# Clustered attention before two feed-forward networks: preparation of the heads rewritten, with copies by DMA and part of the one-hot arithmetic on GpSimd

## The chip, the cores and the metric

One core of a Trainium2 chip runs the whole program. The metric is the device time in microseconds, from the first to the last instruction with what the launch puts around it; lower is better. The engines are named as in the profile: PE is TensorE (matmuls), PEld its weight loads, DVE is VectorE, ACT is ScalarE, POOL is GpSimd, SP is SyncE, which here only issues DMAs.

## The reference

Two batches of eight heads, 768 positions of width 64, and 16 cluster centres a head. A query may attend to a key only if both are nearest, by cosine, to the same centre.

```
q_assign = argmax(q_n @ c_n.T);  k_assign = argmax(k_n @ c_n.T)      # first of equal ones
scores   = where(q_assign == k_assign, q @ k.T / 8, -1e9)
attn     = softmax(scores) @ v                                       # 16 heads of 768 x 64
x        = attn, heads side by side                                  # 1536 tokens x 512
h = x @ w1_in;  g = P(h) / (Q(h) + 1e-6);   x2  = g @ w1_out         # P cubic, Q quadratic, 2048 wide
h = x2 @ w2_in; g = h - tanh(h);            out = g @ w2_out
```

Everything is float32. TensorE is fed numbers rounded to a shorter form (F32R), and each product of weight is made of a rounded part (hi) and its rest (lo): hi x hi, hi x lo, lo x hi.

## The kernel before

The 768 queries of a head are six tiles of 128; the sixteen heads give 96 tiles (`TILES`). Each engine has its own list of work, with semaphores between them.

For one tile, in order: `score_tile` (PE, L945) makes 128 x 768 scores in two PSUM banks, in two accumulating parts, ka with qa (the hi and lo halves of q against hi of k) and kb with qb (hi of q against lo of k, and 16 rows that hold the one-hot of the query's cluster against the mask of the key's cluster times a huge number). `row_max` (DVE, L731) takes the largest, `exp_tile` (ACT, L502) the exponential and its sum, `row_sum` and `row_inverse` (DVE, L736 and L743) its inverse, `scale_probs` (POOL, L349) multiplies. `transpose_probs` (PE, L957) turns the tile in six 128 x 128 pieces into two banks (`pt_ps`), `pt_high` (ACT, L509) and `pt_low` (DVE, L749) split it into hi and lo, and `values` (PE, L968) multiplies with v for three tiles at a time (384 queries, a half of a head). ACT copies one half of the result's partitions beside the other (`other_half`, L592), DVE adds (`add_halves`, L831), ACT and POOL make x_hi and x_lo.

Beside it the next heads are prepared. POOL splits q and k into hi and lo (`nat_q`, `nat_k`) and v (`split_v`, L377); `unit` (PE) is a piece of the preparation: three transposes from nq_a, nk or nq_b into the bank pr_ps (L939), or twelve matmuls with the centres (L929, the similarities). There are nine units a head, eight of them transposes, 24 in all: q, k in the order hi and lo, k in the order hi and hi, and q once more with the one-hot beside it. ACT copies each out (L494, L496, L497). DVE turns the similarities into a one-hot (`onehot`, L705 to L725): sum, maximum, equal to the maximum, times a rank, maximum, equal.

The order of the work is written by hand. `section(s, ...)` is six steps, one tile each, and `STEP_UNITS` says which unit goes with which step; a loop (`Fori`) runs over pairs of heads on every engine, with register-valued waits on SP and POOL. Scores run three tiles ahead of the transposes; there are two score buffers and three of probabilities. The first two heads are prepared ahead of the loop (`FIRST_UNITS`). SP issues all DMAs.

The feed-forward networks follow in 96 steps: `hidden(n)` (PE, L1014) and `output(n)` (L1035) of twelve matmuls each, `tile1` or `tile2` on ACT and DVE, `g_low` on POOL (L462). Weights come in chunks of 512 KB, are rounded by ACT (`round_weights`, L519) and split by POOL (L392) or DVE (L777). Chunks 0 to 3 are loaded at the start of the program, 4 and 5 after the last scores, the others when the attention's memory is free. The first three hidden steps stand between the last tiles of the attention.

Of the kernel before, what the change touches and what calls it, by code (L numbers as in the profile page):

```python
# [5 lines left out]
def clustered_attention_then_two_ffns(  # L6
# [32 lines left out]
    PAIRS = HEADS // 2  # L39
    T = S // P  # L40
# [15 lines left out]
    MASK_AT = 96  # L56
    LANES = 4
    TILES = HEADS * T
    DURING = 6
# [14 lines left out]
    with ctx:  # L74
# [32 lines left out]
        raw_v = [sb(attn_mem, f"raw_v{i}", [P, T * D]) for i in range(2)]  # L107
        nq_a = sb(attn_mem, "nq_a", [P, T, 2 * D])
        nq_b = sb(attn_mem, "nq_b", [P, T, MASK_AT + C])
        nk = sb(attn_mem, "nk", [P, T, 3 * D])  # L110
        qa = [sb(attn_mem, f"qa{i}", [P, S], F32R) for i in range(2)]
        qb = [sb(attn_mem, f"qb{i}", [P, S], F32R) for i in range(2)]
        ka = [sb(attn_mem, f"ka{i}", [P, S], F32R) for i in range(2)]
        kb = [sb(attn_mem, f"kb{i}", [P, S], F32R) for i in range(2)]
        v2 = [sb(attn_mem, f"v2_{i}", [P, T, 2 * D], F32R) for i in range(2)]
        probs = [sb(attn_mem, f"probs{i}", [P, S]) for i in range(3)]
# [5 lines left out]
        cq = sb(attn_mem, "cq", [P, HEADS, 2, C], F32R)  # L122
        cent = sb(attn_mem, "cent", [P, D])
        c_st = sb(attn_mem, "c_st", [P, 8])
        c_hl = sb(attn_mem, "c_hl", [P, 2, 2, D])
        rank = sb(attn_mem, "rank", [P, C])
        sim = sb(attn_mem, "sim", [P, 2 * T, C])
        hot = sb(attn_mem, "hot", [P, 2 * T, C])
# [23 lines left out]
        for c in range(PRELOAD, NF):  # L152
# [6 lines left out]
        qk_in = [sem(f"qk_in{i}") for i in range(2)]  # L159
        v_in = [sem(f"v_in{i}") for i in range(2)]  # L160
# [5 lines left out]
        sp_gate, pool_gate = sem("sp_gate"), sem("pool_gate")  # L166
# [4 lines left out]
        part_done, x_hi_done = sem("part_done"), sem("x_hi_done")  # L171

        max_done, rinv_done, pt_lo_done = sem("max_done"), sem("rinv_done"), sem("pt_lo_done")
        sim_read, onehot_done, xf_done, dve_chain = sem("sim_read"), sem("onehot_done"), sem("xf_done"), sem("dve_chain")

        probs_scaled, natq_done, nat_done, nqb_done, v_split = sem("probs_scaled"), sem("natq_done"), sem("nat_done"), sem("nqb_done"), sem("v_split")
# [21 lines left out]
        UNITS = 9  # L198
        COPIED = (1, 2, 3, 4, 4, 5, 6, 8, 10)
        COPIES = COPIED[-1]  # L200

        STEP_UNITS = {1: (None, 7, None), 2: (8, None, None), 3: (0, 1, None), 4: (2, 3, 4), 5: (None, 5, None),
                      6: (6, None, None)}

        def step_units(t, finish_next, begin_next):
            return [u if u is not None and (finish_next if u >= 7 else begin_next) else None
# [903 lines left out]
```

## Time and profile before

| | us |
|---|---|
| median of the runs (3, from 861.51 to 861.92) | 861.63 |
| the profiled execution | 861.45 |
| its span | 859.6 |
| busy in the span: PE / PEld | 819.1 / 697.7 |
| busy in the span: DVE / ACT / POOL | 548.9 / 540.6 / 349.4 |
| chain that ended last: PE, DVE, ACT, issue | 75%, 10%, 9%, 4% |

Busy time of PE is modelled and its matmuls overlap, so its load is better read from the distance between the starts of two groups. The page says of the 40 slices of 21.5 us:

```
PE   4899999999999989799999999999999999999998
DVE  3788888888888887999887778896611111111111
ACT  4688888888888887788776677777622222222221
POOL 4457576666757583222222222223732222222222
```

The attention is the first 15 slices, the first network ends near the 27th; a digit is the busy share in tenths.

### The profile page before, as it was taken

The page shows a single profiled execution, that of the slowest core. Times are in us where ns is not written, and L with a number is a line of the kernel's source. Part 1 is how long each engine was busy: PE and PEld are TensorE (multiplying, and loading weights), DVE is VectorE, ACT ScalarE, POOL GpSimd, SP SyncE. Part 2 cuts the span into 40 slices and gives each one's busy share as a digit, 9 for nine tenths or more (in the row PEclk, how much of TensorE's full clock was granted, in tenths as well). Part 3 has the DMA queues.
Part 4 walks back from the last instruction along what each step waited for, and adds up shares of the span by engine and source line. Part 5 has one row for each costly group of instructions (what it writes and reads, how often), then busy time and mean ns, then how long its engine had stood idle before and what let it go on. Part 6 is the DMA issues. An engine that isn't in the chain of part 4 may idle for free.

```text
span 859.6 us, 13071 instructions
## 1 busy us (share of the span) xinstructions
PE 819.1 (95%) x4226; PEld 697.7 (81%) x4226; DVE 548.9 (64%) x1016; ACT 540.6 (63%) x1037; POOL 349.4 (41%) x383
## 2 busy tenths in 40 slices
PE   4899999999999989799999999999999999999998
PEld 4888888888888878688888888888888888888886
DVE  3788888888888887999887778896611111111111
ACT  4688888888888887788776677777622222222221
POOL 4457576666757583222222222223732222222222
PEclk9699999999999999999999999999999999999999
DMA  6000100000010010520000002112400010001001
GB/s 200 2 29 29 55 28 27 27 28 27 27 47 18 0 42 8 172 74 1 0 1 1 1 0 74 50 50 83 138 1 1 1 50 1 1 0 50 1 1 49
DMA packets 30618, 29.94 MB, mean 35 GB/s; under 512 B 2416, under 2 KB 24944, under 8 KB 30576
## 3 DMA queue, kind: packets, MB, share of 16 engines
q1 hardware_dynamic: 30576, 29.40, 10.8%
q8 instruction: 24, 0.39, 0.2%
q14 instruction: 18, 0.15, 0.1%
HBM read 26.25 MB, written 3.15 MB: 34 GB/s over the span
## 4 chain that ended last, share of the span: by engine, by line
PE 75%; DVE 10%; ACT 9%; issue 4%; POOL 0%; ACTq 0%; DMA 0%; DVEq 0%
PE y_ps L1035 29%; PE h_ps L1014 29%; PE pv_ps L968 4%; PE pt_ps L957 4%; PE pr_ps L939 3%; PE s_ps L945 3%; ACT probs L502 2%; PE pr_ps L929 2%; ACT pt_hi L509 2%; DVE nmax L731 2%; ACT kb L497 1%; DVE hot L712 1%; DVE xf L831 1%; DVE pt_lo L749 1%; ACT qb L496 1%
## 5 line engine op out<-in xcount | busy, mean ns | idle before, releaser
L462 POOL TENSOR_TENSOR g_lo<-f_t,g_hi 128x512 fp32r<-128x512 f32 x96 | 125.0, 1302 | 381.4 <-ACT g_hi L545 381.4
L884 DVE TENSOR_TENSOR f_t<-h_ps,f_a 128x512 f32<-128x512 f32 x48 | 33.2, 691 | 203.4 <-ACT f_a L644 203.4
L1014 PE MATMUL h_ps<-x_hi,w_hi 128*128 128x512 f32 x384 | 150.3, 391 | 4.4 <-DVE w_lo L777 4.4
L1014 PE MATMUL h_ps<-x_hi,w_lo 128*128 128x512 f32 x384 | 149.9, 390 | 0.0
L1014 PE MATMUL h_ps<-x_lo,w_hi 128*128 128x512 f32 x384 | 149.9, 390 | 0.0
L545 ACT ACTIVATE g_hi<-f_t 128x512 fp32r<-128x512 f32 x96 | 60.8, 633 | 138.2 <-PE y_ps L1035 126.3
L349 POOL TENSOR_SCALAR probs<-probs,rinv 128x768 f32<-128x768 f32 x96 | 87.1, 907 | 110.1 <-DVE rinv L743 110.1
L749 DVE TENSOR_TENSOR pt_lo<-pt_ps,pt_hi 128x384 fp32r<-128x384 f32 x192 | 100.4, 551 | 29.9 <-ACT pt_hi L509 25.8
L509 ACT ACTIVATE pt_hi<-pt_ps 128x384 fp32r<-128x384 f32 x192 | 84.9, 491 | 38.6 <-PE pt_ps L957 37.6
L731 DVE TENSOR_REDUCE nmax<-s_ps 128x1 f32<-128x768 f32 x96 | 90.9, 947 | 7.4 <-PE s_ps L945 7.4
L957 PE MATMUL pt_ps<-ident,probs 128*128 128x128 f32 x576 | 85.2, 283 | 6.8 <-POOL probs L349 5.2
L502 ACT ACTIVATE probs<-s_ps,nmax 128x768 f32<-128x768 f32 x96 | 87.0, 907 | 3.1 <-DVE nmax L731 2.7
L1014 PEld LDWEIGHTS h_ps<-x_hi,w_hi 128*128 128x128 f32 x384 | 72.4, 189 | 20.2 <-DVE w_lo L777 5.2
L1014 PEld LDWEIGHTS h_ps<-x_hi,w_lo 128*128 128x128 f32 x384 | 72.5, 189 | 15.0
L1014 PEld LDWEIGHTS h_ps<-x_lo,w_hi 128*128 128x128 f32 x384 | 72.3, 188 | 15.0
L644 ACT ACTIVATE f_a<-h_ps 128x512 f32<-128x512 f32 x48 | 28.7, 598 | 83.8 <-PE h_ps L1014 83.2
L957 PEld LDWEIGHTS pt_ps<-ident,probs 128*128 128x128 f32 x576 | 65.7, 143 | 17.3 <-DVE pt_lo L749 10.7
L1035 PE MATMUL y_ps<-g_hi,w_hi 128*128 128x512 f32 x192 | 74.8, 390 | 0.8 <-DVE xf L831 0.8
L1035 PE MATMUL y_ps<-g_hi,w_lo 128*128 128x512 f32 x192 | 74.7, 389 | 0.0
L1035 PE MATMUL y_ps<-g_lo,w_hi 128*128 128x512 f32 x192 | 74.7, 389 | 0.0
L1035 PE MATMUL y_ps<-w_hi,g_hi 128*128 128x512 f32 x192 | 74.7, 389 | 0.0
L1035 PE MATMUL y_ps<-w_lo,g_hi 128*128 128x512 f32 x192 | 74.7, 389 | 0.0
(120 smaller groups left out, 1675.6 us busy)
## 6 DMA issues: line engine op xcount, KB each, us to landing
w_raw<-in_moe_w_in_dram SPq DMA_DIRECT2D x32, 256.0 KB, 2.9
w_raw<-in_moe_w_out_dram SPq DMA_DIRECT2D x32, 256.0 KB, 3.2
raw_q<-in_q_dram SPq DMA_DIRECT2D x16, 192.0 KB, 2.6
raw_k<-in_k_dram SPq DMA_DIRECT2D x16, 192.0 KB, 2.7
raw_v<-in_v_dram SPq DMA_DIRECT2D x16, 192.0 KB, 2.4
out_dram<-f_bc SPq DMA_DIRECT2D x12, 256.0 KB, 2.1
cent<-in_centroids_dram SPq DMA_DIRECT2D x1, 32.0 KB, 1.9
coef_raw<-in_moe_a_dram SPq DMA_DIRECT2D x1, 2.0 KB, 3.7
```

The lines of the kernel that those rows point to most:

```text
L349: return pool.tensor_scalar(dst, src, factor, 1.0, ALU.mult, ALU.mult)
L462: pool.tensor_tensor(g_lo[n % 2][:, :], f_t[n % 2][:, :], g_hi[n % 2][:, :].bitcast(F32), ALU.subtract).then_inc(g_lo_done, 1)
L502: act.activation(probs[buf][:, :].rearrange("p (a c) -> p a c", a=2), s_ps[s_buf][:, :, 0:HALF], ACT.Exp, bias=nmax[:, col:col + 1], accum ...
L509: act.activation(pt_hi[tq // HT][:, HT * h2:HT * h2 + HT, (tq % HT) * P:(tq % HT + 1) * P], pt_ps[h2][:, 0:HALF].rearrange("p (c q) -> p c ...
L545: act.activation(g_hi[n % 2][:, :], f_t[n % 2][:, :], ACT.Copy).then_inc(g_hi_done, 1)
L731: dve.tensor_reduce(nmax[:, col:col + 1], s_ps[s_buf][:, :, 0:HALF], AX.XY, ALU.max, negate=True).then_inc(max_done, 1)
L749: dve.tensor_tensor(pt_lo[tq // HT][at], pt_ps[h2][:, 0:HALF].rearrange("p (c q) -> p c q", c=HT), pt_hi[tq // HT][at].bitcast(F32), ALU.s ...
L884: dve.tensor_tensor(f_t[n % 2][:, :], h_ps[n % 4][:, :], f_a[n % 2][:, :], ALU.subtract).then_inc(g_done, 1)
L957: last = pe.transpose(pt_ps[h2][:, i * P:(i + 1) * P], probs[buf][:, c * P:(c + 1) * P], ident[:, :])
L968: last = pe.matmul(pv_ps[:, 0:HALF], v2[par][:, c, :], part[half][:, c, :], start=(c == 0 and part is pt_hi), stop=(c == T - 1 and part is ...
L1014: last = pe.matmul(h_ps[n % 4][:, :], w[f][:, ws], x[:, cols], start=(kt == 0 and i == 0), stop=(kt == KT - 1 and i == 2))
L1035: last = pe.matmul(y_ps[m][:, :], weights, moving, start=(f == 0 and i == 0), stop=(f == NF - 1 and i == 2))
```

## The change

The attention is rewritten; the networks keep their arithmetic. The parts:

- q and k are split into hi and lo once each (nq, nk: 128 wide a tile), and four units of three transposes (Q0, Q1, K0, K1) turn them. One more unit, HOT, turns the one-hots of q and k with two transposes, 96 rows each. SIM is the twelve matmuls with the centres. That is 14 transposes a head instead of 24.
- What another row range or another buffer needs is copied by DMA from SBUF to SBUF, on SP's queue: `spread_q` (one of 64 x 768), `spread_k` (two), `spread_hot` (six of 16 x 256). The scores of a head wait for these (`dup_in`, `hot_in`). qa, ka and qk_b have three buffers.
- Of the one-hot arithmetic DVE keeps the sum and the two maxima; POOL does the rest (`rank_hot`, `finish_hot`) with subtraction, a multiplication by 2^120 and maxima with constants. For the first two heads DVE does all of it.
- The row sums and inverses are made for two tiles at once; POOL scales two tiles one after the other. Scores run four tiles ahead (`LOOK`), and there are four buffers of probabilities.
- No loops: all 96 tiles are written out on every engine, and all waits are on constants. The units stand at fixed steps before their head (`UNIT_STEP`).
- Three heads instead of two are turned ahead of the first scores; at the start ACT and DVE share the rounding and copying. The weights of chunks 0 to 3 are issued after the first heads' copies.
- At the end chunks 0 to 4 are rounded and split at other steps, chunks 4 to 6 are loaded after the last scores, and from chunk 6 on each is rounded and split one step of the network earlier. hidden(3) stands after the last tile.

```diff
     W = 2 * DM
     SCALE = 1.0 / 8.0
     BIG = 2.0 ** 100
-    MASK_AT = 96
+    HUGE = 2.0 ** 120
+    QK_BUFS = 3
+    LOOK = 4
+    PROBS = 4
     LANES = 4
     TILES = HEADS * T
-    DURING = 6
+    DURING = 7
     AHEAD = 3
     PRELOAD = 4
     assert D == 64 and T == 6 and KT == 4 and HALF == 384 and C == 16 and H * C == P
...
+        nq = sb(attn_mem, "nq", [P, T, 2 * D])
+        nk = sb(attn_mem, "nk", [P, T, 2 * D])
+        hot_nat = sb(attn_mem, "hot_nat", [P, 2, T * C])
+        hot_t = sb(attn_mem, "hot_t", [P, 2, P], F32R)
...
+        qa = [sb(attn_mem, f"qa{i}", [P, S], F32R) for i in range(QK_BUFS)]
+        ka = [sb(attn_mem, f"ka{i}", [P, S], F32R) for i in range(QK_BUFS)]
+        qk_b = [sb(attn_mem, f"qk_b{i}", [P, 2, S], F32R) for i in range(QK_BUFS)]
...
+        Q0, Q1, K0, K1, SIM, HOT = range(6)
+        FIRST = 2
+        FIRST_UNITS = [(0, Q0, "s0a"), (0, Q1, "s0b"), (0, K0, "s1a"), (0, K1, "s1b"), (0, SIM, "pv"),
+                       (1, Q0, "pt0"), (1, Q1, "pt1"), (1, K0, "pr"), (1, K1, "s0b"), (0, HOT, "s0a"),
+                       (1, SIM, "pv"), (2, Q0, "pt0"), (2, Q1, "pt1"), (2, K0, "pr"), (2, K1, "s1b")]
+        UNIT_STEP = {HOT: -7, SIM: -13, Q0: -17, Q1: -16, K0: -15, K1: -14}
+        ON_DVE = ((0, Q1), (0, K1))
+
...
+        ACT_CHUNK_AT = {79: 0, 82: 1, 84: 2, 88: 3, 94: 4}
+        POOL_CHUNK_AT = {80: 0, 84: 1, 86: 2, 90: 3}
...
-        ROUND_AT = {n: [n + 3] for n in range(3, NF - 3)}
+        ROUND_AT = {n: [n + 4] for n in range(3, NF - 4)}
...
-        DVE_SPLIT_AT = {c - 2: c for c in range(PRELOAD + 2, NF)}
+        DVE_SPLIT_AT = {c - 3: c for c in range(PRELOAD + 2, NF)}
...
+            def spread_q(g):
+
+                wait_copied(sp, g, Q0)
+                wait_copied(sp, g, Q1)
+                sp.dma_start(qk_b[g % QK_BUFS][0:D, 0, :].bitcast(F32),
+                             qa[g % QK_BUFS][0:D, :].bitcast(F32)).then_inc(dup_in[g % QK_BUFS], 16)
+
+            def spread_k(g):
+
+                wait_copied(sp, g, K0)
+                wait_copied(sp, g, K1)
+                for rows in (slice(0, D), slice(D, 2 * D)):
+                    sp.dma_start(ka[g % QK_BUFS][rows, :].bitcast(F32),
+                                 qk_b[g % QK_BUFS][D:2 * D, 1, :].bitcast(F32)).then_inc(dup_in[g % QK_BUFS], 16)
+
+            def spread_hot(g):
+
+                sp.wait_ge(prep_done, prepared(g, SIM))
+                sp.wait_ge(dup_in[g % QK_BUFS], 48 * (g // QK_BUFS + 1))
+                wait_copied(sp, g, HOT)
+                for c in range(T):
+                    sp.dma_start(qk_b[g % QK_BUFS][D:D + C, :, c * P:(c + 1) * P].bitcast(F32),
+                                 hot_t[c * C:(c + 1) * C, :, :].bitcast(F32)).then_inc(hot_in[g % QK_BUFS], 16)
+
...
+            for k in range(-1, TILES):
+                for g, u in units_at[k]:
+                    if u == Q1:
+                        spread_q(g)
+                    if u == K1:
+                        spread_k(g)
+                    if u == HOT:
+                        spread_hot(g)
+                if (k + 18) % T == 0 and 4 <= (k + 18) // T + 1 < HEADS:
+                    g = (k + 18) // T + 1
+                    sp.wait_ge(q_split, g - 1)
+                    load_q(g)
+                if (k + 15) % T == 0 and 4 <= (k + 15) // T + 1 < HEADS:
+                    g = (k + 15) // T + 1
+                    sp.wait_ge(k_split, g - 2)
+                    load_k(g)
+                if (k + 2) % T == 0 and 2 <= (k + 2) // T + 1 < HEADS:
+                    g = (k + 2) // T + 1
+                    sp.wait_ge(v_split, g)
+                    load_v(g)
...
+            sp.wait_ge(v_split, HEADS)
             for c in range(PRELOAD, DURING):
                 load_weights(c)
-            sp.wait_ge(x_lo_done, 2 * PAIRS + 1)
+            sp.wait_ge(x_lo_done, 2 * PAIRS)
...
+            def split_q(g):
+
+                pool.wait_ge(q_in[g % 2], 16 * (g // 2 + 1))
+                if g > 0:
+                    pool.wait_ge(prep_done, prepared(g - 1, Q1))
+                src = raw_q[g % 2][:, :].rearrange("p (t d) -> p t d", t=T)
+                link(hi_of(nq[:, :, 0:D].bitcast(F32R), src))
+                pool.tensor_tensor(nq[:, :, D:2 * D], src, nq[:, :, 0:D], ALU.subtract).then_inc(q_split, 1)
...
+            def rank_hot(g):
+
+                pool.wait_ge(top_done, g - FIRST + 1)
+                link(pool.tensor_tensor(hot[:, :, :], sim[:, :, :],
+                                        top[:, :].unsqueeze(2).broadcast_to([P, 2 * T, C]), ALU.subtract))
+                link(pool.tensor_scalar(hot[:, :, :], hot[:, :, :], HUGE, -2.0 * C, ALU.mult, ALU.max))
+                pool.tensor_tensor(hot[:, :, :], hot[:, :, :], rank[:, :].unsqueeze(1).broadcast_to([P, 2 * T, C]),
+                                   ALU.add).then_inc(hot_ranked, 1)
+
+            def finish_hot(g):
+
+                pool.wait_ge(top2_done, g - FIRST + 1)
+                pool.wait_ge(prep_done, prepared(g - 1, HOT))
+                link(pool.tensor_tensor(hot_nat[:, :, :].rearrange("p a (t c) -> p (a t) c", c=C), hot[:, :, :],
+                                        top2[:, :].unsqueeze(2).broadcast_to([P, 2 * T, C]), ALU.subtract))
+                pool.tensor_scalar(hot_nat[:, 0, :], hot_nat[:, 0, :], -1.0, 1.0, ALU.max, ALU.add).then_inc(hot_done, 1)
+                pool.tensor_scalar(hot_nat[:, 1, :], hot_nat[:, 1, :], -1.0, BIG, ALU.max, ALU.mult).then_inc(hot_done, 1)
+
...
+            for k in range(TILES):
+                r = k % T
+                if r == 0 and 3 <= (k + 18) // T < HEADS:
+                    split_q((k + 18) // T)
+                if r == 1 and 2 <= (k + 11) // T < HEADS:
+                    rank_hot((k + 11) // T)
+                if r == 2 and 3 <= (k + 16) // T < HEADS:
+                    split_k((k + 16) // T)
+                if r == 3 and 1 <= (k + 3) // T < HEADS:
+                    split_v((k + 3) // T)
+                if r == 4 and 2 <= (k + 8) // T < HEADS:
+                    finish_hot((k + 8) // T)
+                if r == 5:
+                    s = (k - 11) // T
+                    if s >= 1 and s % 2 == 1:
+                        x_low(s // 2, 0)
+                        x_low(s // 2, 1)
+                if k in POOL_CHUNK_AT:
+                    split_weights(POOL_CHUNK_AT[k])
+                if k % 2 == 0 and k + 2 < TILES:
+                    scale_probs(k + 2)
+                    scale_probs(k + 3)
...
+                if u == HOT:
+                    if g > 0:
+                        act.wait_ge(hot_in[(g - 1) % QK_BUFS], 96 * ((g - 1) // QK_BUFS + 1))
+                    act.activation(hot_t[0:T * C, :, :].rearrange("p a x -> p (a x)"), bank[0:T * C, 0:2 * P],
+                                   ACT.Copy).then_inc(prep_copied, 1)
                 else:
...
+            for k in range(TILES):
+                r = k % T
+                if k % HT == 0 and k >= T:
+                    other_half(k // HT - 2)
+                    act.wait_ge(pv_done, k // HT - 1)
+                pt_high(k, 0)
+                pt_high(k, 1)
+                for g, u in units_at[k]:
+                    if u == HOT:
+                        copy_unit(g, u)
+                if k + 3 < TILES:
+                    exp_tile(k + 3)
+                for g, u in units_at[k]:
+                    if u not in (HOT, SIM):
+                        copy_unit(g, u)
+                s = k // T - 1
+                if s >= 1 and s % 2 == 1 and r in (1, 4):
+                    copy_x(s // 2, (0 if r == 1 else 1))
...
+                if k in ACT_CHUNK_AT:
+                    round_weights(ACT_CHUNK_AT[k])
+                if k == TILES - 2:
+                    act.wait_ge(cent_dve, 3)
+                    tile1(0)
+            other_half(HALVES - 2)
+            round_weights(PRELOAD + 1)
+            tile1(1)
+            copy_x(LAST_PAIR, 0)
+            other_half(HALVES - 1)
+            tile1(2)
...
+            def row_inverse(m, count):
+                cols = slice(m % 12, m % 12 + count)
+                dve.wait_ge(exp_done, m + count)
+                link(dve.tensor_scalar(rsum_e[:, cols], rsum[:, cols], 1e-9, None, ALU.add))
+                dve.reciprocal(rinv[:, cols], rsum_e[:, cols]).then_inc(rinv_done, count)
...
+            for k in range(TILES):
+                r = k % T
+                if k % HT == 0 and k >= T:
+                    add_halves(k // HT - 2)
+                pt_low(k, 0)
+                if r == 0 and 2 <= (k + 12) // T < HEADS:
+                    read_top((k + 12) // T)
+                pt_low(k, 1)
+                if r == 3 and 2 <= (k + 9) // T < HEADS:
+                    read_top2((k + 9) // T)
+                if k + LOOK < TILES:
+                    row_max(k + LOOK)
+                if k % 2 == 0 and k + 2 < TILES:
+                    row_inverse(k + 2, 2)
+                if r == 5 and 2 <= (k + 13) // T < HEADS:
+                    read_sim((k + 13) // T)
...
+                if k == TILES - 2:
+                    dve.wait_ge(cent_act, 4)
+                    dve.wait_ge(cent_dve, 3)
+                    tile1(0)
+            add_halves(HALVES - 2)
+            tile1(1)
+            tile1(2)
...
+            for g, u in first[:2]:
+                unit(g, u)
...
+            wait_copied(pe, 0, HOT)
+            wait_copied(pe, 1, K1)
+            score_tile(0)
+            wait_copied(pe, 2, K1)
+            score_tile(1)
+            score_tile(2)
+            unit(1, HOT)
+            score_tile(3)
+            unit(2, SIM)
...
+            for k in range(TILES):
+                transpose_probs(k)
+                for g, u in units_at[k]:
+                    if u != SIM:
+                        unit(g, u)
+                if k + LOOK < TILES:
+                    score_tile(k + LOOK)
+                if k >= HT:
+                    values(k)
+                for g, u in units_at[k]:
+                    if u == SIM:
+                        unit(g, u)
+                if k >= TILES - 3:
+                    pe.wait_ge(exp_done, TILES - (1 if k < TILES - 1 else 0))
+                    hidden(k - (TILES - 3))
+            hidden(3)
+            for k in range(TILES, TILES + HT):
+                values(k)
```

## Rows read from the trace of the kernel before

**Rows 1.** Busy us of PE, PEld, DVE, ACT, POOL; clock; DMA share, GB/s (windows).
```profile
0.00:20.00 20.00, 8.41 (x51) 7.38 (x52) 7.64 (x21) 9.35 (x23) 9.35 (x35) 0.97 0.70 215
...
140.84:159.69 18.85, 17.79 (x123) 15.91 (x122) 16.34 (x40) 16.55 (x39) 13.33 (x17) 1.00 0.10 31
```

**Rows 2.** TensorE in order of time, one head: start, duration, group.
```profile
142.65 0.82 PE L957 MATMUL pt_ps<-ident,probs 128*128 128x128 f32 x6
143.22 0.59 PE L945 MATMUL s_ps<-ka,qa 128*128 128x384 f32 x2
...
155.54 0.55 PE L939 MATMUL pr_ps<-ident,nk 128*128 128x128 f32 x3
155.84 0.60 PE L945 MATMUL s_ps<-ka,qa 128*128 128x384 f32 x2
...
156.62 0.34 PE L968 MATMUL pv_ps<-pt_hi,v 128*128 128x384 f32 x1
...
157.33 0.73 PE L929 MATMUL pr_ps<-cq,qa 128*128 x6
...
158.59 0.87 PE L957 MATMUL pt_ps<-ident,probs 128*128 128x128 f32 x6
```

**Rows 3.** Waits, 60 to 300 us: in total, times, longest.
```profile
POOL probs L349 <- DVE rinv L743: 82.5, 64, 2.5
...
PEld pv_ps L968 <- issue: 5.4, 7, 0.8
```

**Rows 4.** Instructions of that head: busy us, mean ns, idle before.
```profile
L743 DVE RECIPROCAL rinv<-rsum_e 128x1 f32<-128x1 f32 x6 | 1.0, 164 | 0.2
L494 ACT ACTIVATE ka<-pr_ps 128x384 fp32r<-128x384 f32 x2 | 1.0, 491 | 0.0
L497 ACT ACTIVATE kb<-pr_ps 16x384 fp32r<-16x384 f32 x2 | 1.0, 484 | 0.0
...
L736 DVE TENSOR_SCALAR rsum_e<-rsum 128x1 f32<-128x1 f32 x6 | 0.8, 141 | 0.0
...
L712 DVE TENSOR_TENSOR hot<-sim,top 128x192 f32<-128x192 f32 x1 | 0.8, 780 | 0.0
...
L349 POOL TENSOR_SCALAR nq_b<-nq_a 128x384 fp32r<-128x384 f32 x1 | 0.5, 513 | 0.0
...
L722 DVE TENSOR_TENSOR nq_b<-hot,top 128x96 f32<-128x96 f32 x1 | 0.4, 353 | 0.0
...
L716 DVE TENSOR_TENSOR hot<-hot,rank 128x192 f32<-128x192 f32 x1 | 0.3, 342 | 0.0
L725 DVE TENSOR_TENSOR nq_b<-hot,top 128x96 f32<-128x96 f32 x1 | 0.2, 244 | 0.0
```

**Rows 5.** GpSimd's wider operations: of the page, then of 40 to 320 us.
```profile
L462 POOL TENSOR_TENSOR g_lo<-f_t,g_hi 128x512 fp32r<-128x512 f32 x96 | 125.0, 1302 | 381.4 <-ACT g_hi L545 381.4
...
L349 POOL TENSOR_SCALAR probs<-probs,rinv 128x768 f32<-128x768 f32 x96 | 87.1, 907 | 110.1 <-DVE rinv L743 110.1
...
L392 POOL TENSOR_TENSOR w_lo<-w_raw,w_hi 128x1024 fp32r<-128x1024 f32 x3 | 7.1, 2370 | 0.0
```

**Rows 6.** Loads of q: issue in ns, min/median/max; landing after it.
```profile
L284 SPq DMA_DIRECT2D raw_q<-in_q_dram x16: 332/333/432, 1.2 to 255.9; - x16
...
DMA to landing us min/median/max: 2.4/2.6/5.2
```

**Rows 7.** TensorE at the start of the attention.
```profile
38.99 0.90 PE L957 MATMUL pt_ps<-ident,probs 128*128 128x128 f32 x6
```

**Rows 8.** TensorE's last tiles; a wait after them; a piece of the chain.
```profile
290.37 0.87 PE L957 MATMUL pt_ps<-ident,probs 128*128 128x128 f32 x6
...
318.85 0.89 PE L957 MATMUL pt_ps<-ident,probs 128*128 128x128 f32 x6
...
PE h_ps L1014 <- DVE w_lo L777: 4.4, 2, 3.1
...
357.04 4.37 PE h_ps L1014 x12
```

More of the change, by code:

```diff
@@ L158, in clustered_attention_then_two_ffns @@
         small_in, coef_in = sem("small_in"), sem("coef_in")
[L159 to L160 removed]
+        q_in = [sem(f"q_in{i}") for i in range(2)]
+        k_in = [sem(f"k_in{i}") for i in range(2)]
+        v_in = sem("v_in")
+        dup_in = [sem(f"dup_in{i}") for i in range(QK_BUFS)]
+        hot_in = [sem(f"hot_in{i}") for i in range(QK_BUFS)]
         w_in_sem = [sem(f"w_in{i}") for i in range(LANES)]
@@ new lines, in clustered_attention_then_two_ffns @@
+        units_at = {k: [(g, u) for u in UNIT_STEP for g in range(HEADS)
+                        if T * g + UNIT_STEP[u] == k and (g, u) not in first] for k in range(-1, TILES)}
+        unit_order = first + [gu for k in range(-1, TILES) for gu in units_at[k]]
+        copy_order = [gu for gu in unit_order if gu[1] != SIM and gu not in ON_DVE]
+        unit_bank = {(g, u): b for g, u, b in FIRST_UNITS}
+        bank_before, last_in = {}, {"pr": "cent"}
+        for gu in unit_order:
+            bank = unit_bank.setdefault(gu, "pr")
+            bank_before[gu] = last_in.get(bank)
+            last_in[bank] = gu
@@ L457, in _ @@
-            section(HEADS - 1, LAST_PAIR, 1, False, False, True, {2: [2], 3: [3]})
+            split_q(0)
+            split_q(1)
+            split_k(1)
+            split_v(0)
+            split_q(2)
+            split_k(2)
+            for m in range(2):
+                scale_probs(m)
+            for k in range(TILES):
[20 more added lines that the diff above has]
+                    scale_probs(k + 3)
@@ new lines, in score_tile @@
+            def score_tile(m):
+                g = m // T
+                b = g % QK_BUFS
+                if m % T == 0:
+                    wait_copied(pe, g, K1)
+                    pe.wait_ge(dup_in[b], 48 * (g // QK_BUFS + 1))
+                    pe.wait_ge(hot_in[b], 96 * (g // QK_BUFS + 1))
+                if m >= 2:
+                    pe.wait_ge(exp_done, m - 1)
+                cols = slice((m % T) * P, (m % T + 1) * P)
+                for part in range(2):
+                    for half in range(2):
+                        keys = slice(half * HALF, (half + 1) * HALF)
+                        if part == 0:
+                            weights, moving = qa[b][:, cols], ka[b][:, keys]
+                        else:
+                            weights, moving = qk_b[b][0:D + C, 0, cols], qk_b[b][0:D + C, 1, keys]
+                        last = pe.matmul(s_ps[m % 2][:, half, 0:HALF], weights, moving,
+                                         start=(part == 0), stop=(part == 1))
+                last.then_inc(scores_done, 1)
```

724 lines of the change are left out of this document (256 added, 468 removed).

## The prediction

> **What bounds the kernel now.** I read the 40 slices of the page first (under the profile before). The two feed-forward networks, from about 340 us to the end, keep TensorE busy without a gap, and the change touches only their first tiles. The question is therefore the attention, and there I read one head in the steady loop, from one transposed first half of pt to the same point one head on. It takes 18.85 us, in which DVE is busy 16.34, ACT 16.55 and POOL 13.33 us [rows 1]. TensorE's records overlap, so its own load has to be read from the distances between starts: six transposes of probabilities 0.57 us, three preparing transposes 0.30 to 0.33, the four score matmuls 0.78, four value matmuls 0.71, the twelve similarity matmuls 1.26 [rows 2]. A head of before is 6 x (0.57 + 0.78 + 0.71) + 8 x 0.32 + 1.26 = 16.2 us. So no engine fills 18.85: three engines at 16.2 to 16.6 us hand work to each other with little slack, and the remaining 2.3 us is waiting. POOL waits 82.5 us for the inverse row sum between 60 and 300 us, so it comes late because DVE does, not because it is full; and seven waits of TensorE for nothing that the profile shows, 5.4 us, fit the back edges of its loop, about 0.4 us a head [rows 3].
>
> **The change part by part, one head.**
> TensorE: 10 of 24 preparing transposes go, at 0.107 us each: 16.2 - 1.07 = 15.1 us.
> ACT: two ka copies, two qb copies and two 16-row kb copies go, about 0.49 us each [rows 4] (qb taken as the 16-row kb); one copy of the one-hot, 96 x 256, comes. It costs between nothing and another 0.49 us; I take 0.4. 16.55 - 2.9 + 0.4 = 14.0.
> DVE: four one-hot operations go (0.78 + 0.34 + 0.35 + 0.24 = 1.7 us), and the row sum and inverse are done for two tiles at once, half of 0.8 + 1.0 [rows 4]: 16.34 - 1.7 - 0.9 = 13.7.
> POOL: the second halves of q and k and the copy for nq_b go, three operations of 0.51 us [rows 4]: 13.33 - 1.5 = 11.8. It receives six: three subtractions or additions 192 wide, one scalar operation 192 wide and two 96 wide. No such shape is in the trace. From 512 to 1024 wide a two-input operation goes from 1.30 to 2.37 us, 2.1 ns an element; a scalar operation goes from 0.51 at 384 to 0.907 us at 768, 1.0 ns an element [rows 5, 4]. Extended down: 3 x 0.63 + 0.31 + 2 x 0.21 = 2.6 us, with the waits between them 2.9. The lower bound is 1.7, what the four cost on DVE, the upper one 6 x 1.30 = 7.8, each as dear as a 512-wide one. I take 2.9, because the slopes are straight over the widths that are shown: POOL 14.7 us.
> The page "GPSIMD Engine Reference" of the Trainium skill (section "Elementwise — side-by-side cycle accounting") puts data-dependent branching at about 12 cycles an element, where a plain loop takes 1 to 2.6; if the new scalar operations that take a maximum run that way, their 384 elements are some 3.8 us by an estimate from that page's figures instead of 0.7. No row shows a maximum on POOL, so this stands as a rival below.
> Loops: the 0.4 us a head of back edges goes; it is part of the waiting, not of the loads.
>
> Now the waits, which decide how far above 15.1 us the head lands. TensorE's steps are, with r the tile within the head: r = 0 2.06 us; r = 1 to 4 with one unit each 2.38; r = 5 with the one-hot (0.21) and the similarity 3.53. DVE at r = 0 has add_halves 0.56, pt_low twice 0.94, read_top 0.35, row_max 0.87 and the pair's inverse 0.37 = 3.1 us, and can't begin before ACT has copied the other half, 0.7 into the step. The inverse is there at 3.8, the scaled tile at 4.7, and TensorE wants it at 2.06 + 2.38 = 4.4: stall 0.3. POOL then has from 3.8 the two scalings 1.8, rank_hot 1.6 and split_k 1.55, so the tile of r = 4 is scaled at about 9.7 where 9.2 plus the first shift is wanted: 0.2. Then the second scaling, split_v 1.55 and finish_hot 1.1 end at 13.3; TensorE stands before the one-hot transposes at 12.2 + 0.5: 0.6, and ACT, whose one-hot copy stands ahead of exp_tile, waits with it. A few tenths come from value matmuls that want xf. 15.1 + 1.3 = 16.4 us a head. With no such stall it is 15.1; nothing in the schedule makes it less.
>
> The copies by DMA: per head SP issues 3 loads, 3 copies of 196 KB and 6 of 16 KB. An issue takes 0.33 to 0.43 us [rows 6], so twelve are under 5.2 of 16 us. The one-hot's own path is six issues, 2.3 us, then the landing. Loads land in 2.4 to 5.2 us [rows 6]. From the one-hot copy at r = 5 to score_tile of the next head at r = 2 TensorE has about 7.5 us of other work; 2.3 + 2.6 fits, 2.3 + 5.2 just does. I cost it at nothing; if every landing took the 5.2, it would be 0.3 us a head, 4 us in all. The page "DMA: Bandwidth & Descriptors" of the Trainium skill (section "Anatomy of one DMA — SWDGE (gpsimd) path") gives a fixed part of about 2.0 us for a transfer on another path than SP's; by it the one-hot would be hidden with 3 us to spare. No row of before shows a copy from SBUF to SBUF.
>
> Start: until the first scores both kernels need one head prepared and its one-hot. The first head now also goes through six DMAs (about 4.5 us more), while k, q and the copies are spread over ACT and DVE and the similarity stands 2.5 us sooner; the first probabilities are transposed at about 25.5 us as before. Before, the second one-hot then held DVE and TensorE, and tile 3's transposes start at 38.99 [rows 7]; now it lies ahead of the scores. But eight weight loads of 256 KB now stand on SP's queue ahead of the second head's one-hot; at the 215 GB/s of the first 20 us [rows 1] they last 9.8 us from about 21 on, so tile 6's scores come at about 33 and tile 3's transposes at about 37: -2 us, with -6 (no such queue) and +4 as the ends.
>
> Steady part: tile 3 to tile 83 took 290.37 - 38.99 = 251.4 us [rows 7, 8], 3.14 a tile; 80 x 16.4 / 6 = 218.7: -32.7. The last ten tiles took 28.5 us to 318.85 [rows 8]; there are no units left and POOL carries four weight splits of 2.4 us, so I take 25: -3.5, with 0 and -6 as ends. Then the change-over: TensorE stood 4.4 us for w_lo, and the twelve matmuls from 357.04 took 4.37 us [rows 8], where the pace of the score matmuls gives 0.78 / 4 x 512 / 384 x 12 = 3.1. Chunk 6 is now loaded, rounded and split a tile earlier; what is late next is g of the fourth tile, some 0.8 us, and DVE's arithmetic stays full: -4, with 0 and -6 as ends.
>
> Sum against the profiled execution (span 859.6, itself 861.45 us): 861.45 - 2 - 32.7 - 3.5 - 4 = 819.3; that execution lies 0.2 us under the median of the runs, so 819 us.
>
> **Rivals.**
> A, the waits vanish: four probability buffers and one more tile of scores ahead let TensorE run at its load. 15.3 us a head; 251.4 - 204 = -47; with the other terms 861 - 57 = 804 us. For it: POOL's waits show it had room. Against: DVE's late inverse at r = 0 is in the program's order. 0.17.
> B, POOL becomes the bound: the scalar operations with a maximum cost three times 1.3 us instead of 0.7 together, so 14.7 + 3.2 = 17.9 us a head. 251.4 - 238.7 = -12.7, and with POOL full the other terms give less, -1 - 2 - 3: 842 us. For it: POOL is already within half a microsecond of TensorE. Against: the straight slopes. By the skill's rule on branching POOL would come to about 17.8, the same case. 0.15.
> C, the other side: the six one-hot operations on POOL each cost what a 512-wide one does or more, 1.30 us [rows 5]. Their price is then 7.8, POOL is 11.8 + 7.8 + 0.5 for waits = 20.1 us a head, scaled probabilities come late at every tile, and it is 80 / 6 x 1.25 = +17 with the gains at the change-over left, -3: 875 us. It decides from about 19.1 us a head, that is 1.2 us an operation. Against: nothing in POOL's rows is so dear at this width. 0.07.
> D, nothing to be measured: what is saved is lost to a head that lands between, 18.5 to 19. 0.01.
>
> **How the numbers follow.** The forecast, 15.8 to 17.1 us a head, 811 to 829 us, has 0.60. The range reaches to A and B: 803 to 842 us, which leaves C, the slower part of B and the faster end of A out. A measurement of this kernel tells about 0.2% (1.7 us) from no change. Faster by more: 0.60 + 0.17 + 0.15 = 0.92; within: 0.01; slower: 0.07.
>
> **What would show it.** The distance between one head's similarity reductions and the next: 16.4, against 15.3 (A), 17.9 (B), 20 (C). POOL's busy share a head, and the length of its 192- and 96-wide operations (0.63, 0.31, 0.21). TensorE's waits at the one-hot transposes, and at r = 2 and 4 for scaled probabilities. Tile 3 at 37, tile 83 at 256, tile 93 at 281 us. No wait for w_lo of more than 1 us after the attention. The time from the last copy of a one-hot to its landing, under 7.5 us. I am wrong in the mechanism if TensorE waits mainly for hot_in or dup_in, and in the size if POOL's new operations don't lie on the slopes.

## The result and the profile after

The changed kernel takes 838.71 us (median of 4 runs, 838.29 to 838.88) against 861.57 for the one before: ratio 0.9737, 95% interval 0.972 to 0.9754. It is 23 us faster; the forecast of 819 was 20 us too low, and the time lies inside the range given. The profiled execution took 838.88 us, its span is 837.1.

One head first: busy time of each engine over two heads of the changed kernel, then its waits from 60 to 300 us (total, times, longest), as in [rows 1, 3].

```profile
121.14:156.07 34.93, 31.94 (x222) 29.72 (x222) 28.29 (x59) 27.72 (x64) 28.57 (x39) 1.00 0.30 75
```

```profile
POOL probs L407 <- DVE rinv L789: 36.3, 29, 3.4
...
PE pr_ps L953 <- POOL nk L424: 16.7, 12, 1.4
...
PEld pv_ps L1004 <- issue: 6.0, 10, 2.8
...
PE pv_ps L1004 <- DVE xf L805: 3.7, 3, 2.5
...
PE pt_ps L987 <- POOL probs L407: 1.3, 3, 0.9
```

A head takes 17.46 us (18.85 before, 16.4 forecast). Per head TensorE is busy 15.97, DVE 14.1, ACT 13.9, POOL 14.3 us; the loads forecast for the last three were 13.7, 14.0 and 14.7, so they were nearly right and no engine is full. The row that matters is the second: twelve times, once in nearly every head of the window, TensorE stands 1.39 us for nk, the split k of a later head. This wait is not in the prediction.

The places by which the prediction wanted to be judged, TensorE in order of time ([rows 7, 8] of before):

```profile
31.91 1.54 PE L987 MATMUL pt_ps<-ident,probs 128*128 128x128 f32 x6
...
40.59 0.59 PE L974 MATMUL s_ps<-ka,qa 128*128 128x384 f32 x2 [1.47 <-ACT qa L551]
...
41.37 0.82 PE L987 MATMUL pt_ps<-ident,probs 128*128 128x128 f32 x6
...
274.37 0.81 PE L987 MATMUL pt_ps<-ident,probs 128*128 128x128 f32 x6
...
300.10 0.92 PE L987 MATMUL pt_ps<-ident,probs 128*128 128x128 f32 x6 [0.24 <-DVE pt_lo L795]
```

Tile 3 starts at 41.37 (forecast 37), tile 83 at 274.37 (256), tile 93 at 300.10 (281). By stretch, measured against forecast: start +2.4 for -2; tiles 3 to 83 233.0 us for 218.7; last ten 25.7 for 25; from tile 93 to the end 3.8 us less than before, for 4 less. The misses are 4.4 + 14.3 + 0.7 + 0.2 = 19.6 us: 819.3 + 19.6 = 838.9.

Why TensorE waits for nk is read from the chain of waits over one head (start, duration, what), from one similarity reduction to the next:

```profile
156.07 0.03 DVE sim L748
...
156.54 0.54 DVE xf L805
157.09 0.52 DVE pt_lo L795
157.60 0.26 DVE top L754
157.86 0.47 DVE pt_lo L795
158.33 0.86 DVE nmax L782
...
159.37 0.18 DVE rinv L789
...
159.63 1.80 POOL probs L407 x2
161.43 0.49 POOL hot L439
...
162.00 0.86 POOL hot L441
...
162.95 0.59 POOL hot L442
163.54 0.51 POOL nk L407
...
164.13 1.01 POOL nk L424
165.13 0.14 issue
165.27 0.52 PE pr_ps L953 x3
...
170.24 0.11 issue
170.35 0.40 PE pr_ps L943 x2
...
172.15 1.26 PE pr_ps L934 x12
173.41 0.02 issue
173.44 0.56 DVE sim L748
```

It is a closed ring: sim to the inverse 3.5 us on DVE, probabilities, ranking and the split of k 5.5 us on POOL without a pause, then 8.2 us of TensorE to the next sim. 3.5 + 5.5 + 8.2 and the hand-overs make 17.4, and every engine is idle somewhere in that time. TensorE also stands a few tenths before the one-hots' transposes at 170.35, a second deadline behind the first. POOL's new operations, 60 to 260 us (count, total, mean ns):

```profile
L441 POOL TENSOR_SCALAR hot<-hot 128x192 f32<-128x192 f32 x11 | 9.5, 862 | 1.0
L442 POOL TENSOR_TENSOR hot<-hot,rank 128x192 f32<-128x192 f32 x11 | 6.5, 594 | 0.9
L451 POOL TENSOR_SCALAR hot_nat<-hot_nat 128x96 f32<-128x96 f32 x12 | 6.5, 543 | 1.1
L452 POOL TENSOR_SCALAR hot_nat<-hot_nat 128x96 f32<-128x96 f32 x12 | 6.4, 537 | 0.9
L449 POOL TENSOR_TENSOR hot_nat<-hot,top 128x192 f32<-128x192 f32 x12 | 6.2, 515 | 0.0
...
L439 POOL TENSOR_TENSOR hot<-sim,top 128x192 f32<-128x192 f32 x11 | 5.6, 513 | 0.0
```

The three two-input ones are shorter than forecast (0.51 to 0.59 for 0.63), the three with a maximum far longer (0.86 for 0.31, 0.54 for 0.21): together 3.56 us for 2.6.

### The profile page after: what moved, and what is told of

It is laid out like the page before. It is cut to its first block, busy times and chain, and to the rows that moved or that the text cites. A ratio compares the mean times of both kernels' runs of the same rounds, so it can differ in the third digit from the quotient of the medians.

```text
span 837.1 us, 11654 instructions
## 1 busy us (share of the span) xinstructions
PE 794.2 (95%) x4066; PEld 681.7 (81%) x4066; DVE 519.9 (62%) x868; ACT 503.0 (60%) x954; POOL 374.1 (45%) x419
## 4 chain that ended last, share of the span: by engine, by line
PE 66%; DVE 17%; POOL 10%; ACT 3%; issue 2%; DMA 1%; SPq 0%; DVEq 0%; POOLq 0%; ACTq 0%
PE y_ps L1068 26%; PE h_ps L1047 25%; PE s_ps L974 4%; POOL probs L407 4%; PE pv_ps L1004 3%; PE pt_ps L987 2%; PE pr_ps L934 2%; DVE pt_lo L795 2%; DVE nmax L782 2%; DVE f_bc L848 2%; DVE f_t L867 2%; DVE w_lo L822 2%; DVE f_bc L865 2%; DVE f_a L861 1%; POOL nk L424 1%
```

## The experiments

Each experiment changes the kernel after unless it says otherwise. The measured times stand beside 838.71; the runs of the kernel before in the three groups had medians of 860.66, 861.47 and 861.2, so ratios are to those. The head's length is the mean distance of the similarity reductions over ten or eleven heads. It is the better measure for small effects: the first similarity reduction alone starts at about 10.9 us in some profiles and at 12.2 in others.

**1. GpSimd's order** (a1_k_first)

```diff
-  if r == 1: rank_hot(head + 2)    if r == 2: split_k(head + 3)
+  if r == 1: split_k(head + 3)     if r == 2: rank_hot(head + 2)
```

> The changed kernel with two pieces of GpSimd's list exchanged: k is split at the tile with r = 1 and rank_hot stands at r = 2 (before, the other way round). In the changed kernel a head takes 17.4 us, and TensorE stands 1.39 us a head before the transposes of k, for GpSimd's k split. Theory Queue: GpSimd works without a pause from DVE's inverse at r = 0 (159.6) to the end of finish_hot (170.2), 10.6 us, and TensorE's one-hot unit starts right behind that; with DVE's 3.6 and TensorE's 3.1 up to the next similarity this is a closed ring of 17.3 us, which the exchange leaves as long as it is. The wait before k goes and comes back before the one-hot or before a scaled tile: 17.2 to 17.4 us a head, total 0 to -3 us, 836 to 839. Theory Order: the k split is simply late in the list; with the wait gone a head takes 16.1 to 16.3 us: 13 heads x 1.2, total about 823.

838.68 us, ratio 0.9746 (0.9729 to 0.9763): nothing. The wait for nk is gone. In its place TensorE waits one microsecond in each head, two units later, and 6.6 us in all for scaled probabilities (1.3 before the exchange):

```profile
PE pr_ps L943 <- POOL hot_nat L452: 13.1, 13, 1.1
```

The order alone is not the cause; the two deadlines share one stretch of POOL.

**2. Without the maxima** (a2_no_max; the thresholds and one-hots are then not computed)

```diff
-  tensor_scalar(hot, hot, HUGE, -2.0 * C, mult, max)
+  tensor_scalar(hot, hot, 1.0, 1.0, mult, mult)
   # and the two of hot_nat in the same way
```

> The changed kernel with the three scalar operations of GpSimd's one-hot arithmetic as multiplications by 1 in place of their maxima (the one-hots, and so the masks, aren't computed; everything else is as it was). The maxima take 0.86 us at 192 wide and 0.54 us at 96 wide, where the slope of the plain ones gives 0.31 and 0.21. Theory Queue: they shorten to about 0.3 and 0.2, GpSimd's stretch from the inverse to the one-hot shrinks by 1.2 us, and a head with it: 16.2 us, total -16, about 823. Theory Order: only the 0.55 us of the first one lie ahead of the k split, so a head gains 0.55: total -7, about 832. Rival Width: a narrow operation on GpSimd costs what these cost whatever it computes; then nothing changes, 838 to 839.

826.55 us, ratio 0.9602 (0.9581 to 0.9622): 12.2 us less.

```profile
L441 POOL TENSOR_SCALAR hot<-hot 128x192 f32<-128x192 f32 x12 | 4.2, 352 | 1.1
L452 POOL TENSOR_SCALAR hot_nat<-hot_nat 128x96 f32<-128x96 f32 x12 | 3.3, 274 | 0.0
```

Without a maximum the operations do lie near the prediction's slopes (0.35 for 0.31, 0.27 for 0.21); the maximum costs 0.51 and twice 0.27 us more. The head goes to 16.68 us, by 0.8: 0.51 for the operation that stands ahead of nk, and 0.3 because the wait for the one-hots goes too.

**3. One-element row sums** (a3_one_wide)

```diff
-  rsum_e[:, c:c+2] = rsum[:, c:c+2] + 1e-9
+  for each of the two columns: rsum_e[:, c:c+1] = rsum[:, c:c+1] + 1e-9
```

In the kernel after, one such addition takes 2.36 us, exactly beside a weight split on POOL (order of time):

```profile
268.25 2.35 POOL L466 TENSOR_TENSOR w_lo<-w_raw,w_hi 128x1024 fp32r<-128x1024 f32 x1
268.28 2.36 DVE L788 TENSOR_SCALAR rsum_e<-rsum 128x2 f32<-128x2 f32 x1
...
271.53 0.41 PE L1004 MATMUL pv_ps<-pt_hi,v 128*128 128x384 f32 x1 [2.54 <-DVE xf L805]
```

> The changed kernel with DVE's row sums of two tiles made by two operations of one element instead of one of two elements; the inverses stay together. Two elements wide, the operation once took 2.36 us (268.28) and once 0.96 us, exactly beside a GpSimd operation, against 0.16 in the median; one element wide it never took over 0.153 us in the kernel before. Theory Port: from two elements on DVE runs it in a form that needs the port that it shares with GpSimd; one wide, the two long ones go, and with them TensorE's waits of 2.54 us for xf at 271.5: total -2 to -4 us, 835 to 837. Rival: the long ones are waits for something else that one-wide operations have too: no change or +0.5 us for the extra operation.

839.12 us, ratio 0.9744 (0.9728 to 0.9761): no gain, though the longest addition fell from 2357 to 154 ns. The blocking is shown: in this run the two one-column additions at 269.37 take 0.21 us together, beside a weight split that runs for 2.39 us from 269.36. Its price here is next to nothing: from the last similarity reduction to the end this profile is 0.25 us shorter, and the head is 0.06 us longer (17.52), for the second addition stands in the ring.

**4. The kernel before without loops** (b1_unrolled_before)

```diff
-  with X.Fori(a, b) as i:
+  for i in range(a, b):
```

> The kernel before with its five loops over pairs of heads written out, nothing else. It prices the part 'no loops' by itself. Theory Back edge: seven waits of TensorE for nothing that the profile shows, 5.4 us, are the loop's back edges; they go, and a pair of heads takes 37.0 to 37.3 instead of 37.7 us: total -3 to -6 us, 856 to 859. Rival Hidden: the back edges lie beside other engines' waits, a head stays at 18.85 us: within 1 us of before.

858.99 us against 860.66, ratio 0.9978 (0.9969 to 0.9988). A head goes from 18.85 to 18.70. And the wait that I had put down to back edges is still there, and longer:

```profile
PEld pv_ps L968 <- issue: 8.3, 13, 0.7
```

So the loops were worth 1.7 to 1.9 us in all, and the seven waits of [rows 3] were not their back edges.

**5. Weight loads later** (c1_weights_later)

```diff
   # SyncE, before the tiles
-  coefficients; load_weights(0 to 3)
   spread_hot(1)
+  coefficients; load_weights(0 to 3)
```

> The kernel after, with the coefficient and weight loads of the start (8 issues on SyncE, 26.8 to 32.0 us) put behind the one-hot copies of the second head. Theory Start: the copy of the second head's one-hots is issued five microseconds earlier, the 1.47 us wait of TensorE at 40.59 goes, and the program ends 1.5 to 3 us earlier (836 to 837.5). Rival: that wait is hidden work's time, the queue on TensorE at the low clock sets the first head's probabilities, and the time stays within 1 us of 838.7.

837.99 us, ratio 0.9722 (0.9696 to 0.9749): within 1 us, as the rival had it. The wait of 1.47 us at 40.59 goes, and tile 3 stands at 38.88 instead of 41.37; but then:

```profile
41.73 0.85 PE L954 MATMUL pr_ps<-ident,nk 128*128 128x128 f32 x3 [1.93 <-POOL nk L425]
```

2.5 us gained before the first nk are waited off at it, and the fifth head's similarity reduction starts at 68.54 instead of 68.67. About 1 us of the 2.5 is not the wait but TensorE's clock: the six transposes of the second tile take 1.05 us here and 1.48 in the changed kernel.

**6. The inverse first** (d1_inverse_first: VectorE's order in a head)

```diff
   pt_low(k, 0)
-  read_top(head + 2)
   pt_low(k, 1)
+  row_inverse(k + 2, 2)
   row_max(k + LOOK)
-  row_inverse(k + 2, 2)
+  read_top(head + 2)
```

> The kernel after, with VectorE's order in a head changed: the inverse of the row sums before the next row maximum (0.87 us) and before the read of the top coefficients (0.26 us). GpSimd waits for that inverse in each head. Theory Ring: the closed chain sim, inverse, probabilities, one-hots, split of k, transposes, sim gets 1.1 us shorter, so a head takes 16.3 to 16.5 us in place of 17.46 and the whole about 825 (12 to 15 us less). Rival Busy: GpSimd or TensorE is occupied anyway and the gain is under 4 us.

827.47 us, ratio 0.9601 (0.9575 to 0.9628): 11.2 us less, with no operation added or removed. A head takes 16.59 us, 0.87 less, the length of the row maximum; the 0.26 of the read did not come in addition, because the inverse now waits for ScalarE's last probabilities (DVE rsum_e for ACT probs, 8.7 us in 36). TensorE's wait for nk is halved (7.5 us in 11) and not gone. This is what the ring foretells, seen from VectorE's side; experiment 8 tests it on TensorE's.

**7. The clamp on ScalarE** (e1_clamp_on_act)

```diff
   # GpSimd
-  hot_nat = hot - top2;  half 0: max(-1) + 1;  half 1: max(-1) * BIG
+  hot_nat = hot - top2
   # ScalarE, in the copy of the transposed one-hots out of PSUM
-  Copy
+  Relu(x + 1);  half 1: BIG * x - BIG
```

> The kernel after, with GpSimd's two maximum operations of each head from the third on left out and the same clamp done on ScalarE, in the copy out of PSUM that it does anyway and one more operation on one half. GpSimd loses about 1.1 us a head, ScalarE gains about 0.3. Theory Queue (what delays the split of k is GpSimd's stretch without a pause): like the kernel without maxima, 12 to 16 us less, about 825. Rival Act: the clamp's second operation on ScalarE lands in the same ring and gives half of it back, about 832.

835.63 us, ratio 0.9694 (0.9668 to 0.9721): 3.1 us less, neither theory's number. The intervals of the two ratios touch, but the head is shorter too (17.25 for 17.47). The wait for nk is as before:

```profile
PE pr_ps L961 <- POOL nk L425: 16.4, 12, 1.4
```

What it frees on POOL lies behind nk, so only the short wait for the one-hots goes. "POOL's stretch without a pause" was too coarse: what counts is what lies ahead of the next thing wanted.

**8. Transposes doubled on either side of the wait** (h1_q_twice; h2_k_twice with K0, K1)

```diff
-  for i in range(HT):  transpose(bank[i], ...)
+  for i in (range(HT) twice, if head >= 3 and u in (Q0, Q1)):  transpose(bank[i], ...)
```

> The kernel after, with the six transposes of a head's q done twice for the heads from the fourth on (+0.66 us of TensorE a head, the result unchanged). They stand between sim and TensorE's wait for nk, where TensorE has 1.4 us to spare. Theory Ring: the wait for nk shrinks from 1.39 to about 0.7 us and the head stays at 17.46, the whole within 1.5 us of 838.7. Rival Share (every microsecond of TensorE's work counts, whatever its place): 13 heads by 0.66, about 847.

> The same with the six transposes of k in place of q's. They stand behind the wait for nk, on the stretch that leads to the next sim. Theory Ring: a head takes 0.5 to 0.66 us longer (0.3 of it may be hidden by the wait for the one-hots), the whole 843 to 847. Rival Share: about 847 as for q. If q costs nothing and k costs all, the place decides; if both cost the same, the ring is no more than a picture.

q twice: 838.88 us, ratio 0.9748 (0.9723 to 0.9772), head 17.46. k twice: 842.78, ratio 0.9802 (0.9771 to 0.9833), head 17.85, which is 0.39 more. The expectation had said that up to 0.3 of the 0.66 us would be hidden by the wait for the one-hots, and 0.27 are missing; no run isolates that part. TensorE's wait for nk in the one with q twice:

```profile
PE pr_ps L953 <- POOL nk L424: 10.5, 12, 0.9
```

The same 78 transposes cost nothing ahead of the wait and 4 us behind it.

**9. All edits together, with and without the clamp on ScalarE** (f1_all: the diffs of 1, 5, 6 and 7, and the one below; g1_all_but_act: without 7)

```diff
   score_tile(3)
-  unit(2, SIM)
   transpose_probs(0)
+  unit(2, SIM)
```

> All of it together: weights later, inverse first, clamp on ScalarE, split of k before the ranking, and the third head's first one-hot product behind the transposes of the first tile. Theory Ring: the chain gets some 2.3 us shorter, TensorE's own work of a head (about 15.1 us) becomes the bound, a head takes 15.1 to 15.6 us and the whole 805 to 812. Rival: another wait takes its place near 16.3 us a head, and the whole is 820 to 825.

> All edits together but the clamp on ScalarE: GpSimd keeps the two maximum operations at the end of the one-hots. Without the clamp the one-hots come 1.1 us later, and with the split of k first TensorE would wait for them: theory Two deadlines: a head 0.2 to 0.5 us longer than the 15.95 of all together, 821 to 825. Rival: TensorE is the bound with or without it (its chain there is without a pause) and the time is 818 within 1 us.

f1_all: 818.0 us, ratio 0.9497 (0.9462 to 0.9531), head 15.95. The chain of waits over one head of it:

```profile
by line: PE pv_ps L1014 28.5%; PE pt_ps L997 27.4%; PE s_ps L984 26.9%; PE pr_ps L963 8.3%; PE pr_ps L944 8.3%; PE pr_ps L953 1.4%; issue 0.3%
```

Only TensorE is left in it, but that is not yet its load: a short stall between two of its groups is counted by this view as work of the group behind it (the four value matmuls from 153.41 stand in it with 0.95 us, elsewhere with 0.71). The last two steps of the same head show it:

```profile
154.21 0.82 PE L997 MATMUL pt_ps<-ident,probs 128*128 128x128 f32 x6
...
156.62 0.82 PE L997 MATMUL pt_ps<-ident,probs 128*128 128x128 f32 x6
...
160.22 0.87 PE L997 MATMUL pt_ps<-ident,probs 128*128 128x128 f32 x6
```

A step with one unit takes 2.39 to 2.41 us where nothing holds it (2.38 forecast), the step with the similarity 3.60 (3.53), the first one 2.12 (2.06): 2.12 + 4 x 2.39 + 3.60 = 15.3 us. The step before these takes 2.69, because the value matmuls at 153.41 start late, and between 60 and 300 us TensorE waits 6.5 us in all for xf. So the load is 15.3, and some 0.7 us a head in this version are still short stalls. g1_all_but_act: 824.43 us, ratio 0.9592 (0.9561 to 0.9623), head 16.60, and TensorE waits for the other deadline:

```profile
PE pr_ps L945 <- POOL hot_nat L453: 6.7, 13, 0.7
```

The clamp on ScalarE gives 3.1 us alone and 6.4 in company. By the waits it is the order of experiment 1 that makes the difference: with k split late TensorE stops at nk; with k split early it stops at the one-hots, and those come sooner when POOL has no maxima to do for them. No run has the clamp and the order alone together. The edits of 1, 5, 6 and 7 one by one sum to 15.0 us, together they give 20.7, but with a fifth edit that was never run alone. It acts only at the start, so the stretch from the fifth head's similarity reduction to the last one is the fair comparison: there the four single edits give 0.07, 0.05, 9.66 and 2.46 us, 12.2 in sum, and all together give 16.7.

**10. One-element sums in that version** (g2_all_one_wide: f1_all with the diff of 3)

> All edits together, and the two row sums taken one column at a time, so that no VectorE operation of two elements meets a GpSimd one. With TensorE as the bound its waits for xf (6.5 us in 11 between 60 and 300 us, the longest 2.5) cost the whole: 1 to 4 us less than 818.0. Rival Slack: as in the kernel after, where the same edit gave nothing, no change within 1 us, for it adds 0.1 us a pair of tiles to VectorE.

813.74 us, ratio 0.9467 (0.9435 to 0.9499): the lowest median, 25 us under the changed kernel. Its gain over f1_all is not clear of noise: the two intervals overlap, and the four runs of either kernel spread over more than 4 us. And the reason given holds for less than half of it. The head is 15.97, as long as without it. Of the 5.3 us between the two profiled executions 3.6 are there at the fifth head's similarity reduction (61.37 for 64.94), and 1.9 come after 240 us, where f1_all has two long two-column additions, 1.85 us at 247.59 and 1.36 at 274.94; the waits of TensorE behind them are 2.46 us for xf and 1.17 for pt_lo, where this run has 0.83 and 0.37. Of the first part 0.65 us are there at tile 0's transposes (28.59 for 29.24); the rest arises where TensorE's clock differs, the same window of f1_all and then of g2_all_one_wide, the clock in the third number from the right:

```profile
30.00:35.00 5.00, 5.00 (x24) 4.90 (x23) 2.29 (x6) 1.86 (x4) 3.74 (x5) 0.50 0.10 19
```

```profile
30.00:35.00 5.00, 4.14 (x32) 3.84 (x32) 4.36 (x11) 3.25 (x8) 3.83 (x5) 1.00 0.09 17
```

One runs at 1.2 GHz here, the other at 2.4. In g2_all_one_wide it rises within tile 0's transposes (28.6 us), in f1_all only at about 38, after the same kinds of work. Why it rose sooner was not isolated, so of the 4.3 us between the medians at most some 1.9 can be put down to the edit.

## Why the prediction was right in sign and 20 us too low

**The steady part is the term that failed** (218.7 us, measured 233.0). Its direction and the loads held: 10 transposes less, DVE and ACT relieved, POOL at 14.3 of 14.7 forecast. In POOL's case that was luck. The head that I read of the kernel before had 13.33 us of POOL's work, but heads alternate there, for the two x_lo operations come only in every second one; the head before it shows 11.39:

```profile
121.06:139.92 18.86, 17.86 (x122) 15.95 (x122) 16.32 (x39) 15.81 (x36) 11.39 (x16) 1.00 0.10 31
```

So the base was 1.0 us too high on average, and the new operations 1.0 us too low. The walk through the waits failed at one step. I let POOL do the two scalings, rank_hot and split_k from 3.8 us on, and asked only when the tile of r = 4 is scaled. I did not ask who wants the split k. By my own numbers it was ready at 3.8 + 1.8 + 1.6 + 1.55 = 8.75, and TensorE's unit at r = 3 stands at 2.06 + 2 x 2.38 + 0.57 = 7.4: a stall of 1.35. That 1.39 was measured comes from two errors that cancel: in the head shown above POOL was done 9.25 us after the head's first transposes, 0.5 later than by my numbers because of the maxima, and TensorE stood there at 8.0 instead of 7.4. The stalls I did name were smaller: scaled tiles 1.3 us in all the heads (forecast 0.5 a head), one-hots a few tenths (0.6), xf 3.7 us in all. In sum: 16.4 was 15.1 of load and 1.3 of named stalls; 17.46 is 15.3 of load, 1.39 for nk and 0.8 of all other stalls. Experiments 1, 6 and 8 show that this ring, not an engine's share, sets the head.

**Load of TensorE**: 15.1 forecast, 15.3 by the undisturbed steps of f1_all. Rival A (15.3 a head, all waits gone) was reached by no version: the best head is 15.95 us, with some 0.7 us of short stalls in it. So A had the load right, and the waits did not vanish.

**POOL's new operations**: 2.6 forecast, 3.56 measured. This is the sign that I had named for a wrong size: they don't lie on the slopes. The maxima's own price is 1.05 us by experiment 2, which is worth 12 us of time. Rival B came within 4 us of the measured time (842) with half of its mechanism: maxima are dearer, but POOL is not full. The page "GPSIMD Engine Reference" of the Trainium skill (section "Elementwise — side-by-side cycle accounting") has the direction right if the maximum is such a branch; the estimate from its figures was 3.8 us for the 384 elements, and 1.94 was measured. Rival C, all six at 1.30, fell: the longest is 0.86.

**Start** (-2, measured +2.4). Two steps failed. The one-hots' six copies take 3.93 us to issue at 17.36, not 2.3, for one takes 0.59 us, as the two rows (issue in ns min/median/max; landing) show:

```profile
L325 SPq DMA_DIRECT2D qk_b<-hot_t x96: 586/594/1650, 17.4 to 280.3; - x96
...
DMA to landing us min/median/max: 1.8/1.8/5.2
```

And tile 0's transposes, forecast at 25.5, stand at 31.91, because TensorE first does a score tile, the one-hots and the similarity of the heads behind it, at the lower clock: a pair of its score matmuls takes 0.98 us at 22.65 and 0.59 at 40.59 (the granted clock of this stretch is given as 1.00, but f1_all shows the same 0.98 with 0.50). The kernel before did its first scores at the lower clock too (1.01 us at 19.77), but not all of its preparation: six similarity matmuls take 0.82 us at 12.65 there and 1.44 at 10.67 in the changed kernel. How much of the 4.4 us is the clock no run isolates. The queue of weight loads was real, 26.8 to 32.0 us, and its 1.5 us wait too; experiment 5 shows that removing it gives nothing while the ring stands behind it. So the start's term had its error, and even without it the time would not have followed.

**In the steady part the DMA copies are hidden**, as I had cost them: no wait for them between 60 and 300 us, though the one-hots' path of issues and landing is 3.93 + 1.8 us for the 2.3 + 2.6 forecast. By the page "DMA: Bandwidth & Descriptors" of the Trainium skill (section "Anatomy of one DMA — SWDGE (gpsimd) path") some 2.0 us a transfer were to be expected of that path; on SP's path the 16 KB copies take 1.8.

**Loops**: I gave them 0.4 us a head, read from a wait whose owner the profile does not name. Experiment 4: 0.15 us a head.

**Last ten tiles and change-over**: 25.7 for 25 and -3.8 for -4. The wait for w_lo is 1.3 us where 4.4 stood [rows 8]; I had said not over 1:

```profile
PE h_ps L1047 <- DVE w_lo L822: 1.3, 1, 1.3
```

## What to carry to other kernels

When engines that are each 80 to 90% busy hand work round, find the closed ring and add up its pieces. What is on it counts until the next wait takes over (0.39 of 0.66 us in experiment 8, 0.87 of 1.13 in experiment 6). What is beside it counts nothing as long as a wait absorbs it. Moving VectorE's inverse ahead of its row maximum gave as much as half of the whole rewrite. In a walk through an in-order queue, ask for every item when it is done and when its reader wants it, not only for the items that look critical. Edits to a ring don't add: 12.2 us one by one were 16.7 together, and an edit worth nothing alone can be what lets the next one pay. A view that puts the whole chain on one engine does not show that engine's load: add up its undisturbed steps.

## What the runs showed of the hardware that I had not expected

A scalar operation with a maximum on GpSimd takes 862 ns at 192 elements a partition and 540 at 96, where the same with two multiplications takes 352 and 273: 2.7 ns an element for the maximum. A VectorE addition of two columns was held for as long as GpSimd's two-input operation beside it ran (2.36 us), one of one column never (154 ns at most in 96); beside GpSimd's scalar operation of 0.85 us the one of two columns took 0.31 us (f1_all, 55.81). SyncE takes 0.59 us to issue one of the one-hots' copies from SBUF to SBUF against 0.33 for a load of q in the kernel before [rows 6]. But this is not a price of the copies alone: in the changed kernel the same load of q takes 0.58 us right behind a copy (36.86, 53.01) and 0.33 behind another load (5.32), and that of k 0.44 behind a load (21.96). Why was not isolated. The copies land in 1.8 us (16 KB) and 2.7 to 3.0 us (192 KB).
